# Fewer TensorE waits on GpSimd's transfers in a recurrence followed by an expert layer

## The chip, the cores and the metric

The kernel runs on one core of a Trainium2 chip. The metric is the device time of one execution in microseconds. Before the change three runs took 564.1, 559.63 and 563.5 us, with a median of 563.5 us.

## The reference

Two stages are chained. The first is a gated recurrence over 4 sequences of 5056 steps, with 256 channels each:

```
sig = 1.0 / (1.0 + np.exp(-f_logit))
f = lower_bound + (1.0 - lower_bound) * sig
h = f[:, t] * h + (1 - f[:, t]) * x[:, t]      # for each t; y[:, t] = h
```

The second treats the 20224 rows of y as tokens and sends each to one of 8 experts, the one whose normalized embedding has the largest cosine with the token:

```
logits = xn @ en.T / tau
expert_idx = np.argmax(logits, axis=1)
gate_w = softmax(logits)[chosen expert]
out[mask] = gate_w[mask, None] * (np.maximum(x[mask] @ w1[e], 0.0) @ w2[e])
```

The inner width of an expert is 1024. Input and output are float32, and the kernel multiplies in bf16 inside the experts.

## The kernel before, in words

**Chunks.** The tokens are taken in 40 chunks of 512 (the last has 256). For each chunk SyncE loads f_logit and x (the tiles `fin` and `xin`), TensorE transposes them (L782, L816), ScalarE makes the gate f (L793, L799), and VectorE multiplies (L824) and scans (L840). One or two chunks form a group, of which there are 22. Per group TensorE computes the logits (L945, L949), VectorE finds the expert and the slot of each token, and the rows of h go back to token order in the tile `Yt`.

**Row transfers.** GpSimd then scatters the rows of a group to a buffer in HBM, `XsScratch`, sorted by expert: one indirect transfer for every 128 tokens (`gate_`, L1109), so 4 for a group of one chunk and 8 for a group of two. There are 158 of them.

**Expert tiles.** A tile is 256 rows of one expert (`tile_`). SyncE loads it from `XsScratch`, transposed, into `ys`, and the rows' gates and numbers into `xm`. TensorE multiplies by w1 (L1434, 16 matmuls, two steps of 8) and by w2 (L1482, 16 matmuls, four steps of 4). ScalarE and VectorE apply the ReLU in between (L1455, L1460) and at the end scale the two halves of the result into `osb` (L1497, L1501). GpSimd scatters each half to its place in the output (L1507): 2 output transfers for a tile, 162 for the 81 tiles that run. Ten more tiles stand behind a branch that these inputs don't take. `osb` has 6 buffers, `ys` 6, `Yt` 6 and `xm` 14.

**The order of the work.** Nothing is issued as it is written. `op` records each operation with what it depends on, and `schedule` runs a model of the five engines and fixes the order of each engine's instructions. `resolve` turns dependences into semaphore waits and leaves out those that an engine is already known to have passed. In the model a transfer of GpSimd that is marked `paced` gets one more dependence: the last TensorE step that the model has ended by the time the transfer is issued (`past[-1]`, with `PACE` 0). On the chip GpSimd then waits for that step. All row transfers are marked, and all output transfers but those of the last four tiles. The model also caps the end of a marked transfer at its issue time plus `DMA_FIX`.

GpSimd has one queue of instructions in a fixed order, on which the 16 loads of the expert weights (L762), the row transfers and the output transfers alternate.

Of the kernel before, what the change touches and what calls it, by code (L numbers as in the profile page):

```python
# [34 lines left out]
class Prog:  # L35
# [93 lines left out]
    def schedule(self, first, caps):  # L129
# [43 lines left out]
        while True:  # L173
            best = None
            for e in free:
                while wait[e] and wait[e][0][0] <= free[e]:
                    t, p, i, o = heapq.heappop(wait[e])
                    heapq.heappush(avail[e], (p, i, o))
                if avail[e]:
                    s = free[e]  # L180
                elif wait[e]:
                    s = wait[e][0][0]
# [6 lines left out]
            s, e = best  # L189
# [6 lines left out]
            if soon is not None:  # L196
                wait[e].remove(soon)
                heapq.heapify(wait[e])
                s, p, i, o = soon
            elif avail[e]:  # L200
                p, i, o = heapq.heappop(avail[e])
            else:
                t, p, i, o = heapq.heappop(wait[e])
            gap = s - free[e]
            if e == "pe" and s < self.COLD and gap > self.IDLE:
                room = [(t, q) for q, t in enumerate(frees) if t is not None and t <= s - self.IDLE]
                if room and ready_at(self.warm_on) is not None:
                    t, q = min(room)
                    a = max(t, free[e], ready_at(self.warm_on))
                    n = int((s - a - self.REST) / (self.UNIT * (2 if s < self.COLD else 1)))  # L210
# [29 lines left out]
            if o.dma is not None:  # L240
                bus = max(bus, free[e]) + o.nbytes / self.DMA_RATE
                o.end = max(bus, free[e]) + self.DMA_FIX
                if e == "pool" and o.paced:
                    o.end = min(o.end, free[e] + self.DMA_FIX)
            else:
                o.end = free[e] + self.LAG[e]
# [126 lines left out]
def bass_hgrn_recurrence__then__cosine_router_kernel(  # L373
# [41 lines left out]
    with ExitStack() as es:  # L415
# [106 lines left out]
        def dve(fn, n, fast=False, **k):  # L522
            return op("dve", fn, 75 + n * (0.55 if fast else 1.04), **k)

        def act(fn, n, ptrs=0, **k):
            return op("act", fn, 70 + 0.833 * n + 110 * ptrs, **k)
# [380 lines left out]
        def views(g, hr=None):  # L907
            cc = groups[g]
            K, nb = len(cc), nof(cc[0]) // P
            J = K * nb  # L910
            q = g % R2
            o = bof[g][1] * 8

            def rt_():
                return bank[hr.b][:, 0:392].rearrange("p (b c) -> p b c", b=4)[:, 0:nb, :]

            def Lv():
                return rt_()[:, :, 0:64].rearrange("p b (k e) -> p b k e", k=2)[:, :, 0:K, 0:8]

            def Nv():  # L920
                return rt_()[:, :, 64:98:32][:, :, 0:K]

            def v4(t, o=0):
                return t[:, o * 8 : (o + J) * 8].rearrange("p (b k e) -> p b k e", b=nb, k=K)

            def v3(t, o=0):
                return t[:, o : o + J].rearrange("p (b k) -> p b k", b=nb)

            def bc(t, o=0):
                return v3(t, o).unsqueeze(3).to_broadcast([P, nb, K, 8])  # L930

            return K, nb, J, q, Lv, Nv, v4, v3, bc
# [115 lines left out]
        def gate_(bi):  # L1048

            gg = batches[bi]  # L1050
            JJ = views(gg[0])[2] + (8 if len(gg) > 1 else 0)
            q, y = bi % R2, bi % NY

            n_, y_, t_ = nrm[q][:, 0:JJ], nr2[q][:, 0:JJ], nr3[q][:, 0:JJ]
            ki, ky, kt = ("nrm", q), ("nr2", q), ("nr3", q)
            root(n_, y_, t_, nr4[q][:, 0:JJ], nr5[q][:, 0:JJ], [ki], ky, kt, ("nr4", q), ("nr5", q), 16)
            dve(
                lambda e: e.tensor_scalar(y_, t_, 1e-6, tau, op0=ALU.add, op1=ALU.mult),
                16, r=[kt], w=[ky],
            )  # L1060
            dve(
                lambda e: e.reciprocal(rs[q][:, 0:JJ], nr2[q][:, 0:JJ]), 16,
                r=[("nr2", q)], w=[("rs", q)],
            )
            d3 = df[q][:, 0 : JJ * 8].rearrange("p (j e) -> p j e", e=8)
            dve(
                lambda e: e.tensor_tensor(
                    d3, d3, rs[q][:, 0:JJ].unsqueeze(2).to_broadcast([P, JJ, 8]), ALU.mult
                ),
                128, r=[("rs", q), ("df", q)], w=[("df", q)],  # L1070
            )
            act(
                lambda e: e.activation(exb[q][:, 0:JJ, 0:8], d3, AF.Exp),
                128, r=[("df", q)], w=[("exb", q)],
            )
            dve(
                lambda e: e.tensor_reduce(den[q][:, 0:JJ], exb[q][:, 0:JJ, :], AX.X, ALU.add),
                144, r=[("exb", q)], w=[("den", q)],
            )
            yf = Yt[y][:].bitcast(F32)  # L1080
            for g in gg:
                K, nb, J = views(g)[0:3]
                v3 = views(g)[7]
                o = bof[g][1] * 8
                dve(
                    lambda e, K=K, nb=nb, o=o, v3=v3: e.reciprocal(
                        yf[:, o : o + K * 4, P].rearrange("p (k b) -> p b k", k=K)[:, 0:nb, :],
                        v3(den[q], o),
                    ),
                    8, r=[("den", q)], w=[("Ytg", y)],  # L1090
                )
            K, nb = views(gg[-1])[0:2]
            R = bof[gg[-1]][1] * 8 + (K - 1) * 4 + nb
            dve(
                lambda e: e.tensor_scalar(
                    Yt[y][:].bitcast(I32)[:, 0:R, P + 1], tokf[:, 0:R],
                    float(groups[gg[0]][0] * CH), None, op0=ALU.add,
                ),
                8, r=["tokf"], w=[("Yti", y)], order=[pr.writer[("Ytg", y)]],
            )  # L1100
            for g in gg:
                K, nb, J = views(g)[0:3]
                o = bof[g][1] * 8
                for b in range(nb):
                    for k_ in range(K):
                        j = b * K + k_
                        sc = op(
                            "pool",
                            lambda e, j=o + j, i=o + k_ * 4 + b: e.indirect_dma_start(  # L1109
                                out=Xs[:, :],  # L1110
                                out_offset=bass.IndirectOffsetOnAxis(
                                    ap=sli[y][:, j : j + 1], axis=0
                                ),
                                in_=Yt[y][:].bitcast(I32)[:, i, :],
                                in_offset=None,
                            ),
                            1280, r=[("Yt", y, k_, 0), ("Yt", y, k_, 1), ("Ytg", y), ("Yti", y), ("ytz", y), ("sli", y)],
                            w=[("Xs", g)], dma=f"sc{y}_{k_}", nbytes=100000, chain=False,
                        )
                        sc.paced = True  # L1120


        def update_(u, g, last):
# [188 lines left out]
        NM = N // T + E // 4  # L1312
# [5 lines left out]
        def tile_(j, u, g, n):  # L1318
# [105 lines left out]
            for mp in range(2):  # L1424
# [26 lines left out]
                for m, h in ((2 * mp, hh[0]), (2 * mp + 1, hh[1])):  # L1451
                    o = hT[qh][:, 2 * m : 2 * m + 2, :].rearrange("p f c -> p (f c)")
                    if m % 2 == 0:
                        act(
                            lambda e, o=o, h=h: e.activation(o, bank[h.b][:], AF.Relu), 512,  # L1455
                            h=h, w=[("hT", qh, m)], prio=EVP(pr.prio), tag="mid",
                        )
                    else:
                        dve(
                            lambda e, o=o, h=h: e.tensor_scalar(  # L1460
                                o, bank[h.b][:], 0.0, None, op0=ALU.max
                            ),
# [41 lines left out]
            for s in range(2):  # L1504
                sc = op(
                    "pool",
                    lambda e, s=s: e.indirect_dma_start(  # L1507
                        out=out[:, :],
                        out_offset=bass.IndirectOffsetOnAxis(
                            ap=xm[qx][:, s, 1:2], axis=0  # L1510
                        ),
                        in_=osb[qo][:, s, :],
                        in_offset=None,
                        bounds_check=N - 1,
                        oob_is_err=False,
                    ),
                    1280, r=[("osb", qo, s)] + xk, w=[("out", j, s)], dma=f"od{qo}_{s}",
                    nbytes=170000, prio=OUTP(pr.prio),
                )
                sc.paced = n < NM - 4  # L1520


        last_of = {cc[-1]: g for g, cc in enumerate(groups)}
# [20 lines left out]
        def put(j, n):  # L1544
            u, g = avail[j]
            pr.prio = 10000 + n
            tile_(j, u, g, n)

        for c in range(NCH):
            pr.prio = c  # L1550
            if c >= 2:
                load(c)
            F_(c)
            X_(c)
            Y_(c)
            if c == 0:
                for i in range(2 * E):
                    wload(i, c)
            if c == 1:
                late_constants()  # L1560
            if c in last_of:
                g = last_of[c]
                route_(g)
                bi, gi = bof[g]
                if g == batches[bi][-1]:
                    gate_(bi)
                for u, at in enumerate(ups):
                    if at == g:
                        update_(u, g, u == len(ups) - 1)
# [63 lines left out]
```

How the kernel before makes its waits and increments, by code:

```python
            def part(e, items):  # L347
                for o, waits in items:
                    for key, v in waits:
                        e.wait_ge(sems[key], v)
                    with nc.allow_low_precision(reason="whole numbers below 2**24"):
                        ins = o.fn(e)
                    if o.dma is not None:
                        ins.then_inc(sems[o.dma], 16)
                    elif o.used:
                        ins.then_inc(sems[eng], 1)
```

## Time and profile before

| | |
|---|---|
| runs | 564.1, 559.63, 563.5 us (median 563.5) |
| the profiled execution's own time | 565.46 us |
| its span, first to last instruction | 563.7 us |
| TensorE matmuls | 475.2 us busy, 84% |
| VectorE | 359.5 us, 64% |
| GpSimd | 331.9 us, 59% |
| ScalarE | 321.1 us, 57% |
| mean granted TensorE clock | 0.963 of full speed |

Engines are PE (TensorE matmuls), PEld (TensorE weight loads), DVE (VectorE), ACT (ScalarE), POOL (GpSimd) and SP (SyncE). A line such as L1109 is a line of the kernel. The idle time before an instruction is put down to what ended it; "issue" means that the profile shows nothing that the engine waited for, and "remote" that a semaphore came well after the recorded end of the instruction that sends it. Ends of matmuls are modelled. Landing times of most transfers could not be paired with their issues, so a wait for a landing may appear under another name.

### The profile page before, as it was taken

How to read it: one execution, taken by the hardware profiler on the slowest of the kernel's cores; microseconds unless marked ns; L12 is line 12 of the kernel's file. 1: busy time of each engine (PE TensorE's matmuls, PEld its weight loads, DVE VectorE, ACT ScalarE, POOL GpSimd, SP SyncE). 2: the span in 40 equal slices, each digit the busy share in tenths (PEclk: the TensorE clock that was granted, in tenths of full speed). 3: DMA queues.
4: the chain of work that ended last, by engine and by line, in shares of the span. 5: the costliest groups of instructions: out<-in, count | busy, mean ns of one | idle time of the engine just before them, and what ended most of it. 6: DMA issues, size and time to landing. Idle time of an engine off the chain costs nothing. (4 is left out here: it accounts for less than half of the span.)

```text
span 563.7 us, 12407 instructions
## 1 busy us (share of the span) xinstructions
PE 475.2 (84%) x4106; PEld 382.8 (68%) x4106; DVE 359.5 (64%) x1075; ACT 321.1 (57%) x573; POOL 331.9 (59%) x388
## 2 busy tenths in 40 slices
PE   7796778979798789887887988888988897978994
PEld 4474557757577567656765657777777776867894
DVE  7869978877787667875877876533444343443452
ACT  4878768877787566757776753333333332333342
POOL 6164565655665565564666665656665666655555
PEclk8969988998998889999999999999999999999998
DMA  8999999999999788879896543353343433444422
GB/s 243 302 311 313 318 254 311 287 254 219 206 234 241 202 205 190 238 172 219 221 241 133 117 92 99 113 127 105 100 110 95 110 88 100 106 109 101 106 65 74
DMA packets 119681, 100.49 MB, mean 178 GB/s; under 512 B 96884, under 2 KB 98687, under 8 KB 119616
## 3 DMA queue, kind: packets, MB, share of 16 engines
q1 hardware_dynamic: 101664, 59.38, 42.5%
q0 software_dynamic: 16224, 40.26, 26.2%
q8 instruction: 36, 0.59, 0.5%
q10 hardware_dynamic: 1728, 0.01, 0.2%
q14 instruction: 29, 0.24, 0.2%
HBM read 59.21 MB, written 32.93 MB: 163 GB/s over the span
## 5 line engine op out<-in xcount | busy, mean ns | idle before, releaser
L1507 POOL DMA_INDIRECT out_dram<-osb,xm x162 | 160.7, 992 | 107.6 <-issue 34.0
L1109 POOL DMA_INDIRECT XsScratch<-Yt,sli x158 | 152.2, 963 | 105.6 <-issue 26.6
L1434 PE MATMUL bank<-ys,wall 128*128 128x256 bf16 (+1 forms) x1392 | 174.4, 271 | 19.1 <-issue 13.4
L1482 PE MATMUL bank<-wall,hT 128*128 x1296 | 172.8, 274 | 15.0 <-issue 12.6
L1460 DVE TENSOR_SCALAR hT<-bank 128x512 bf16<-128x512 f32 x162 | 108.4, 684 | 100.8 <-remote 46.0
L1434 PEld LDWEIGHTS bank<-ys,wall 128*128 x1392 | 147.5, 145 | 34.9 <-issue 24.7
L1455 ACT ACTIVATE hT<-bank 128x512 bf16<-128x512 f32 x162 | 94.0, 597 | 114.1 <-remote 49.5
L1482 PEld LDWEIGHTS bank<-wall,hT 128*128 128x128 bf16 x1296 | 124.4, 98 | 42.9 <-issue 23.0
L840 DVE TENSOR_TENSOR_SCAN hb<-fg,hb,bank 128x512 f32<-128x512 f32 (+4 forms) x78 | 95.9, 1236 | 0.1
L1501 DVE TENSOR_SCALAR osb<-bank,xm 128x256 f32<-128x256 f32 x81 | 38.8, 479 | 59.7 <-ACT osb L1497 32.6
L1497 ACT ACTIVATE osb<-bank,xm 128x256 f32<-128x256 f32 x81 | 38.4, 475 | 59.7 <-remote 17.4
L816 PE MATMUL bank<-ident,xin 128*128 128x128 f32 x316 | 53.2, 294 | 22.7 <-ACT fg L799 12.9
L799 ACT ACTIVATE fg<-th,cs 128x512 f32<-128x512 f32 (+1 forms) x80 | 64.4, 812 | 1.4 <-DVE cs L627 0.2
L816 PEld LDWEIGHTS bank<-ident,xin 128*128 128x128 f32 x316 | 37.7, 149 | 34.6 <-ACT fg L799 16.9
L824 DVE SCALAR_TENSOR_TENSOR bank<-fg,bank 128x512 f32<-128x512 f32 (+1 forms) x80 | 54.1, 680 | 9.6 <-PE bank L816 6.8
L793 ACT ACTIVATE th<-bank 128x512 f32<-128x512 f32 (+1 forms) x80 | 46.3, 592 | 22.7 <-PE bank L782 14.2
L782 PE MATMUL bank<-ident,fin 128*128 128x128 f32 x316 | 53.5, 300 | 4.5 <-DMA fin<-in_f_logit_dram 2.0
L782 PEld LDWEIGHTS bank<-ident,fin 128*128 128x128 f32 x316 | 40.4, 155 | 12.2 <-issue 4.5
L852 ACT ACTIVATE sq<-hb 128x1024 f32<-128x1024 f32 (+1 forms) x40 | 41.8, 1045 | 2.0 <-DVE hb L840 1.6
L945 PE MATMUL bank<-hb,eT 128*8 128x512 f32 (+1 forms) x160 | 41.7, 599 | 0.3 <-issue 0.3
L949 PE MATMUL bank<-sq,onesf 128*1 128x512 f32 (+1 forms) x160 | 41.5, 597 | 0.0
L861 ACT ACTIVATE hbf<-hb 128x512 bf16<-128x512 f32 x50 | 31.4, 629 | 4.7 <-DVE hb L840 4.2
(139 smaller groups left out, 305.3 us busy)
## 6 DMA issues: line engine op xcount, KB each, us to landing
fin<-in_f_logit_dram SPq DMA_DIRECT2D x39, 512.0 KB
xin<-in_x_dram SPq DMA_DIRECT2D x39, 512.0 KB
wall<-in_moe_w_dram POOLq DMA_DIRECT2D x16, 512.0 KB, 10.6
out_dram<-osb,xm POOLq DMA_INDIRECT x162
XsScratch<-Yt,sli POOLq DMA_INDIRECT x158
ys<-XsScratch SPq DMA_TRANSPOSE x81
xm<-XsScratch SPq DMA_DIRECT2D x75, 2.0 KB
osb<-XsScratch SPq DMA_DIRECT2D x6, 136.0 KB
```

The source lines that it names most:

```text
L782: i = e.transpose(bank[h.b][:, b : nb * P : nb], fin[q][:, b, dh * P : (dh + 1) * P], ident[:],)
L793: lambda e, dh=dh, h=h: e.activation(th[dh][:, 0:n], bank[h.b][:, 0:n], AF.Tanh, scale=0.5),
L799: lambda e, dh=dh: e.activation(fg[c % 2][:, dh, 0:n], th[dh][:, 0:n], AF.Identity, bias=cs[:, dh, 0:1], scale=cs[:, dh, 1:2],),
L816: i = e.transpose(bank[h.b][:, b : nb * P : nb], xin[q][:, b, dh * P : (dh + 1) * P], ident[:],)
L824: lambda e, dh=dh, h=h: e.scalar_tensor_tensor(out=bank[h.b][:, 0:n], in0=fg[c % 2][:, dh, 0:n], scalar=1.0, in1=bank[h.b][:, 0:n], op0=AL ...
L840: lambda e, dh=dh, s0=s0, s1=s1, init=init, h=h: e.tensor_tensor_scan(hb[c % NH][:, dh, s0:s1], fg[c % 2][:, dh, s0:s1], bank[h.b][:, s0:s ...
L1109: lambda e, j=o + j, i=o + k_ * 4 + b: e.indirect_dma_start(out=Xs[:, :], out_offset=bass.IndirectOffsetOnAxis(ap=sli[y][:, j : j + 1], axis=0
L1434: i = e.matmul(bank[hh[f // 2].b][:, at : at + R_], wall[:, bass.ds(a1[j, s][(4 * mp + f) * DT + kt] - WA - WREV, 2 * FT * P),].bitcast(BF ...
L1455: lambda e, o=o, h=h: e.activation(o, bank[h.b][:], AF.Relu), 512,
L1460: lambda e, o=o, h=h: e.tensor_scalar(o, bank[h.b][:], 0.0, None, op0=ALU.max),
L1482: i = e.matmul(po(s), hT[qh][:, kf, s * P : (s + 1) * P], wall[:, bass.ds(a2[j, s if last else 0][kf] - WA, 2 * D)].bitcast(BF16), start=( ...
L1507: lambda e, s=s: e.indirect_dma_start(out=out[:, :], out_offset=bass.IndirectOffsetOnAxis(ap=xm[qx][:, s, 1:2], axis=0), in_=osb[qo][:, s, :],
```

## The change

Two marks are set for fewer transfers. Of a group's row transfers, only every fourth (`j % 4 == 0`) is paced now; of a tile's two output transfers, only the first (`s == 0`). The cap on the end of a transfer in the model now goes by the name of its semaphore (`sc` for rows, `od` for outputs) instead of the mark, so that it still holds for all of them.

```
-                if e == "pool" and o.paced:
+                if e == "pool" and o.dma[:2] in ("sc", "od"):
                     o.end = min(o.end, free[e] + self.DMA_FIX)
...
-                        sc.paced = True
+                        sc.paced = j % 4 == 0
...
-                sc.paced = n < NM - 4
+                sc.paced = s == 0 and n < NM - 4
```

On every engine the instructions stand in the same order as before; only waits differ. Of the 320 row and output transfers that run, 283 waited for a TensorE semaphore (149 of the 158 row transfers, 134 of the 162 output transfers); now 116 do (40 and 76). Two pieces of GpSimd's queue show it. In brackets are the semaphores that an instruction waits for: `s_pe`, `s_dve` and `s_act` are those of TensorE, VectorE and ScalarE, `s_w8` that of a weight load, `s_xm5` that of a tile's gates. A row with `-` is before, with `+` after.

The first piece is GpSimd's queue in the first 100 us, with row transfers of two groups between weight loads:

```order
 L762 DMA wall<-in_moe_w_dram 128x2x1024 [waits s_w8]
 L1109 DMA XsScratch<-Yt,sli 164096x136 [waits s_pe,s_dve]
-L1109 DMA XsScratch<-Yt,sli 164096x136 [waits s_pe] x3
+L1109 DMA XsScratch<-Yt,sli 164096x136 x3
 L762 DMA wall<-in_moe_w_dram 128x2048 [waits s_w9]
-L1109 DMA XsScratch<-Yt,sli 164096x136 [waits s_pe] x4
+L1109 DMA XsScratch<-Yt,sli 164096x136 [waits s_pe]
+L1109 DMA XsScratch<-Yt,sli 164096x136 x3
 L762 DMA wall<-in_moe_w_dram 128x2x1024 [waits s_w10]
```

The first transfer of four keeps its wait, and the other three follow it without one.

The second piece is GpSimd's queue where tiles and chunks run together, after the change alone:

```order
+L1507 DMA out_dram<-osb,xm 20224x256 [waits s_xm5,s_pe,s_act]
+L1507 DMA out_dram<-osb,xm 20224x256 [waits s_dve]
+L1109 DMA XsScratch<-Yt,sli 164096x136 [waits s_pe]
+L1109 DMA XsScratch<-Yt,sli 164096x136
+L1507 DMA out_dram<-osb,xm 20224x256 [waits s_xm6,s_pe,s_act]
+L1507 DMA out_dram<-osb,xm 20224x256 [waits s_dve]
+L1109 DMA XsScratch<-Yt,sli 164096x136 x2
```

The second output transfer of a tile waits for its data alone (`s_dve`), and of the row transfers one in four waits. The longest run of transfers without a TensorE wait is now 4.

## Rows read from the trace of the kernel before

**Rows 1.** The page: busy time of TensorE and GpSimd, slices, and queue q0.

```profile
PE 475.2 (84%) x4106; PEld 382.8 (68%) x4106; DVE 359.5 (64%) x1075; ACT 321.1 (57%) x573; POOL 331.9 (59%) x388
...
q0 software_dynamic: 16224, 40.26, 26.2%
```

**Rows 2.** Busy time by stage: start to end, busy us (instructions) by engine, clock, DMA, GB/s.

```profile
core 0: us, PE busy (x) PEld busy (x) DVE busy (x) ACT busy (x) POOL busy (x), PEclk, DMA share, GB/s
0.00:100.00 100.00, 77.77 (x586) 56.81 (x590) 82.43 (x279) 74.34 (x119) 54.36 (x104) 0.88 1.01 294
100.00:350.00 250.00, 213.66 (x1876) 165.36 (x1869) 189.71 (x633) 172.25 (x306) 149.70 (x154) 0.97 0.82 198
350.00:553.00 203.00, 180.00 (x1617) 157.54 (x1616) 84.76 (x159) 72.57 (x146) 121.92 (x125) 1.00 0.41 103
```

**Rows 3.** TensorE's waits, whole span: what it waited for, us, times, longest us.

```profile
PE bank L1434 <- issue: 13.4, 29, 2.3
PE bank L816 <- ACT fg L799: 12.9, 10, 2.8
PE bank L1482 <- issue: 12.6, 24, 1.2
...
PE bank L1434 <- DVE osb L1501: 2.4, 3, 1.6
PE bank L816 <- DMA xin<-in_x_dram: 2.0, 1, 2.0
PE bank L782 <- DMA fin<-in_f_logit_dram: 2.0, 3, 1.6
```

**Rows 4.** The groups of both kinds of transfer: busy us, mean ns, idle before.

```profile
L1507 POOL DMA_INDIRECT out_dram<-osb,xm x162 | 160.7, 992 | 107.6 <-issue 34.0 <-DVE hT L1460 26.1 <-ACT osb L1497 7.2
L1109 POOL DMA_INDIRECT XsScratch<-Yt,sli x158 | 152.2, 963 | 105.6 <-issue 26.6 <-PE bank L782 13.1 <-PE bank L1434 13.1
```

**Rows 5.** Line L1109 alone: shortest, median and longest of its transfers in ns.

```profile
L1109 POOL DMA_INDIRECT XsScratch<-Yt,sli x158: 952/959/1059, 27.5 to 482.6; - x158
```

**Rows 6.** Row transfers alone by stage (stretch, POOL busy and count, clock, DMA, GB/s).

```profile
0.00:100.00 100.00, 35.95 (x37) 0.88 1.01 294
100.00:350.00 250.00, 88.36 (x92) 0.97 0.82 198
350.00:553.00 203.00, 27.87 (x29) 1.00 0.41 103
```

**Rows 7.** GpSimd in order of time: start us, us, instruction, idle before it.

```profile
257.18 1.00 POOL L1507 DMA_INDIRECT out_dram<-osb,xm  x1 [0.30 <-issue]
258.48 0.96 POOL L1109 DMA_INDIRECT XsScratch<-Yt,sli  x1 [0.30 <-issue]
259.75 0.95 POOL L1109 DMA_INDIRECT XsScratch<-Yt,sli  x1 [0.30 <-issue]
262.36 0.96 POOL L1109 DMA_INDIRECT XsScratch<-Yt,sli  x1 [1.66 <-PE bank L1434]
263.62 0.95 POOL L1109 DMA_INDIRECT XsScratch<-Yt,sli  x1 [0.30 <-issue]
```

**Rows 8.** SyncE's waits from 350 us on: what it waited for.

```profile
SPq L1329 <- remote: 25.8, 9, 4.3
...
SPq L1329 <- PE bank L1482: 17.5, 9, 2.6
SPq L1329 <- PE bank L1434: 11.7, 6, 3.3
```

**Rows 9.** ScalarE and GpSimd at the end of the span, in order of time.

```profile
552.53 0.48 ACT L1497 ACTIVATE osb<-bank,xm 128x256 f32<-128x256 f32 x1 [2.44 <-PE bank L1434]
...
553.80 0.98 POOL L1507 DMA_INDIRECT out_dram<-osb,xm  x1 [2.27 <-DVE osb L1501]
555.09 0.99 POOL L1507 DMA_INDIRECT out_dram<-osb,xm  x1 [0.30 <-issue]
...
560.26 0.98 POOL L1507 DMA_INDIRECT out_dram<-osb,xm  x1 [0.30 <-issue]
```

**Rows 10.** TensorE's waits from 350 us on.

```profile
PE bank L1482 <- issue: 10.8, 21, 1.2
PE bank L1434 <- issue: 9.8, 24, 1.1
...
PE bank L1434 <- DVE hT L1460: 0.9, 2, 0.5
```

**Rows 11.** GpSimd, then TensorE, around one of these stalls, in order of time.

```profile
465.18 0.99 POOL L1507 DMA_INDIRECT out_dram<-osb,xm  x1 [0.30 <-issue]
466.47 0.98 POOL L1507 DMA_INDIRECT out_dram<-osb,xm  x1 [0.30 <-issue]
468.97 0.96 POOL L1109 DMA_INDIRECT XsScratch<-Yt,sli  x1 [1.51 <-remote]
...
466.32 0.60 PE L1482 MATMUL bank<-wall,hT 128*128 x4
467.32 0.27 PE L1482 MATMUL bank<-wall,hT 128*128 x1 [0.39 <-issue]
468.01 0.38 PE L1482 MATMUL bank<-wall,hT 128*128 x2 [0.43 <-issue]
```

## The prediction

> **What bounds the kernel now.** I read the busy times first, by stage. TensorE's matmuls are busy for 475.2 of 563.7 us, more than any other engine [rows 1], and from 350 us to 553 us for 180.0 of 203.0 us, while VectorE, ScalarE and all transfers are near or under half [rows 2]. The reader should see there that GpSimd is busy for 121.92 us in the same 203 us: it has room.
>
> Next come TensorE's own waits [rows 3]. The largest are stalls with no cause in the profile ("issue", 13.4 and 12.6 us) and 12.9 us for ScalarE's gate in the chunks. Three waits are for anything that a transfer of any queue could carry: 2.0 us for x, 2.0 us for f_logit, and 2.4 us behind VectorE's write of `osb`, a tile that an output transfer frees. No row of TensorE's waits names a row transfer or an output transfer. SyncE, which loads the tiles that the row transfers fill, waits in the late stage for TensorE, 17.5 and 11.7 us [rows 8]; another 25.8 us stand under "remote", a semaphore that came later than the modelled end of its sender. That too is a TensorE signal as far as can be told, and no landing of a row transfer stands in the list.
>
> Then GpSimd itself [rows 4, 7]. A transfer holds it for 0.963 or 0.992 us, and one that is free to go follows the one before after 0.30 us, which is a period of about 1.27 us. Where a wait binds, the gap is longer: 1.66 us before the row transfer at 262.36. So the removed waits do bind now, and not all are empty.
>
> So the bound is TensorE, in the late stage nearly alone, and GpSimd follows it.
>
> **The change part by part.** The order of the instructions stays on all engines, so the change is waits alone: 167 TensorE waits fewer on GpSimd (283 less 116), none added. Nothing is moved past anything.
>
> *What GpSimd gains.* The idle time before row and output transfers is 105.6 + 107.6 = 213.2 us [rows 4]. Of that, 320 x 0.30 = 96 us is the unavoidable gap; the other 117 us or so is waiting, and part of it goes. But the first transfer of four and the first of a tile keep their wait, the longest run without one is 4, and the gap left out is mostly 0.7 to 1.4 us (1.66 less 0.30 at 262.36), so a single transfer starts some 1 to 4 us sooner. It lies beside TensorE's work; if that cover were gone, up to those 117 us would matter.
>
> *What an earlier row transfer is worth.* It would matter if SyncE waited for it. By its waits it does not [rows 8], so I take 0. A gain is left possible all the same, since landings are badly paired in this trace: were a tenth of the 25.8 us under "remote" such waits and TensorE short of that tile, 2.6 us. The ends are 0 and -2.6.
>
> *What an earlier output transfer is worth.* It frees `osb` sooner. The nearest row is TensorE's 2.4 us behind the write of `osb` [rows 3]. The ends are 0 and -2.4 us; I take -1.0, because the write itself, 0.48 us for a half tile [rows 9] in each of the three times, stays.
>
> *The end of the span.* ScalarE's scaling at 552.53 ends at 553.01, the next output transfer starts at 553.80, and five more follow in steps of 1.29 us, to 561.24 [rows 9]. These belong to tiles that were not paced before either. Worth 0; it would take an earlier end of TensorE to move it.
>
> *What the burst costs.* Three of four row transfers now leave sooner than the plan had them, beside the loads of x, f_logit and the tiles. The queue that GpSimd feeds took 26.2% of the 16 engines' span [rows 1], or 147.7 us, for 338 transfers (162, 158, 16 weight loads and 2 small ones), which is 0.44 us each. Three brought forward hold a load behind them for at most 1.3 us. The ends are 0, since TensorE hardly waits for a load, and 13 us, if each of the nine or ten bursts of four in the first 100 us (37 row transfers [rows 6]), where the transfer engines are full (1.01) [rows 2], delayed a load that TensorE then lacks. I take +0.5, close to the low end, because the row nearest to it is the 4.0 us of waits for x and f_logit in the whole span [rows 3], and an eighth more of that is 0.5. The Trainium skill, DMA: Bandwidth & Descriptors, section Issuing engines are not separate DMA queues, says that transfers started by any engine run on the same 16 engines and interleave. By it earlier row transfers must come out of the loads' share; the trace agrees that the engines are full at first (1.01), and this speaks against the change.
>
> *Making descriptors in a burst.* Row transfers take 952 to 1059 ns with a median of 959 over a span in which VectorE is busy 64% [rows 1, 5], so none is stretched to speak of; I take 0. The Trainium skill, SBUF — State Buffer, section SBUF: two separate sides, warns that VectorE in certain modes locks GpSimd out while it writes descriptors, which would stretch a burst. No row here shows it, and by the 1059 ns it could add 0.1 us to a transfer.
>
> *Sum.* 565.46 - 1.0 + 0.5 = 565.0 us against the profiled execution's own time. That execution lies 2.0 us above the median of 563.5, so against the runs the sum gives **563.0 us**, no change that could be measured. A change is told from none here at about 1%, that is below 557.9 or above 569.1; the three runs alone spread over 4.5 us.
>
> **The rivals.**
>
> *Faster: the late stalls belong to GpSimd's timing.* In the last 214 us TensorE loses 10.8 + 9.8 = 20.6 us in 45 stalls with no wait in the program [rows 10], as between 466.32 and 468.01, where matmuls that need nothing come 0.7 us apart [rows 11]. If they come from something that the transfers' timing sets, and an evener stream takes a third away, 6.9 us go: 563.0 - 6.9 = 556.1 us. For it: GpSimd ran several transfers in a row just before (465.18, 466.47) [rows 11]. Against it: GpSimd is held by a stall in TensorE anyway, so the rows would look like this either way, and the stage before 350 us has the same rate of transfers with fewer of these stalls (26.0 us in all, of which 20.6 are late) [rows 3, 10]. Chance 0.16.
>
> *Slower: bursts in the first 100 us.* Place: the chunks up to 100 us, where the transfer engines are full at 1.01 and 294 GB/s and weights are loaded too [rows 2]. Three row transfers go 1 to 3 us earlier, and the load of x or f_logit behind them comes up to 1.3 us later. Price: half of the 13 us above, 6.5 us, 569.5 us. It decides from the point where a load has less than 1.3 us to spare in more than about half of the bursts. For it: the full engines, and four waits for such loads already (4.0 us). Against it: x and f_logit have three buffers each, and TensorE waited only those four times. Chance 0.08.
>
> *Slower: longer stalls late.* The same 45 stalls, longer by a third because output transfers now come in closer pairs: 563.0 + 6.9 = 569.9 us. The evidence is that of the first rival with the other sign. Chance 0.07.
>
> *The change does nothing.* The kept wait, or the data, holds each run of four just as long. The time is 563.5 us; inside the forecast, and not told from it.
>
> **How the numbers follow.** Forecast, including the last case: 0.69; its own range is 559.5 to 567, the spread of the runs shown with the bounds of -2.4 and -2.6 and part of the burst's cost. The faster rival gets 0.16, the two slower ones 0.15. The predicted time is 563.0. To leave out no more than 2 in 10, the range takes in the faster rival at 556.1 and the two slower ones at 569.5 and just short of 569.9: 555.5 to 569.8. Faster by over 1%: 0.16; within 1%: 0.69; slower by over 1%: 0.15.
>
> **What would show it.** In the profile after, GpSimd's busy time stays near 332 us and its gaps before the second to fourth row transfer and before the second output transfer fall to 0.30 us, with longer gaps before the ones that still wait. TensorE's busy time stays near 475 us, its waits for x and f_logit near 4 us, its "issue" stalls after 350 us near 20 us. The last run of six output transfers starts 0.8 us after a scaling and has the same 1.29 us steps. I am wrong if "issue" falls or rises by over 5 us from 350 us on (first and third rival), if waits for x and f_logit pass 8 us (second), or if a wait for a row transfer's landing held TensorE all along without being named.

## The result, and the profile after

The changed kernel took 600.41 us (median of 6 runs, 592.47 to 607.6), the kernel before beside it 561.76 us (6 runs, 559.63 to 564.1). The ratio is 1.0645, with a 95% interval of 1.0586 to 1.0703: **slower by 6.5%**, where no measurable change was forecast. One run of after, 607.6 us, fell in a slower state of the chip and isn't in the ratio, which for that reason lies below that of the two medians.

The profiled execution of after took 599.74 us, its span is 597.9 us, 34.2 us more than before, and the mean granted clock is 0.925 (0.963 before). The page's line of busy times, to be held against [rows 1]:

```profile
PE 494.0 (83%) x4106; PEld 394.4 (66%) x4106; DVE 361.0 (60%) x1075; ACT 325.4 (54%) x573; POOL 332.6 (56%) x388
```

All engines ran the same instructions. GpSimd, VectorE and ScalarE were busy for nearly what they were before, but TensorE's matmuls for 18.8 us longer, and TensorE stood idle for 15.4 us longer (597.9 - 494.0 = 103.9, before 563.7 - 475.2 = 88.5). The two make the 34.2 us.

GpSimd's groups of transfers, the view of [rows 4], and the spread of the row transfers, the view of [rows 5]:

```profile
L1507 POOL DMA_INDIRECT out_dram<-osb,xm x162 | 160.8, 993 | 155.5 <-DVE osb L1501 34.1 <-issue 27.1 <-DVE hT L1460 22.6
L1109 POOL DMA_INDIRECT XsScratch<-Yt,sli x158 | 152.7, 966 | 93.0 <-issue 39.4 <-PE bank L1434 8.6 <-PE bank L782 7.3
```
```profile
L1109 POOL DMA_INDIRECT XsScratch<-Yt,sli x158: 956/962/1072, 26.7 to 514.7; - x158
```

A transfer lasts as long as before. The idle time moved: less before row transfers (93.0 after 105.6), much more before output transfers (155.5 after 107.6). GpSimd reaches them sooner and then waits for data that come later.

TensorE's waits over the whole span, against [rows 3]:

```profile
PE bank L816 <- ACT fg L799: 18.0, 13, 4.0
PE bank L1434 <- issue: 13.4, 25, 1.2
PE bank L1482 <- issue: 10.2, 20, 1.0
PE bank L816 <- issue: 5.9, 5, 3.7
...
PE bank L1434 <- DVE osb L1501: 4.6, 3, 3.7
PE bank L1434 <- DVE hT L1460: 4.2, 5, 2.3
```
```profile
PE bank L816 <- DMA xin<-in_x_dram: 1.2, 1, 1.2
```

The waits for ScalarE and VectorE grew and became longer singly (4.0 us where 2.8 was the longest); those for loads shrank. Something holds up all the compute engines. What it is stands in the waits of ScalarE and VectorE, which the prediction did not read. Before first, two rows of ScalarE and one of VectorE:

```profile
ACT hT L1455 <- remote: 49.5, 13, 5.7
ACT osb L1497 <- remote: 17.4, 6, 5.5
```
```profile
DVE hT L1460 <- remote: 46.0, 14, 5.2
```

The same waits after, with the next row of each engine:

```profile
ACT hT L1455 <- remote: 41.9, 11, 6.6
ACT osb L1497 <- remote: 23.4, 8, 4.3
ACT th L793 <- remote: 13.4, 4, 5.4
```
```profile
DVE hT L1460 <- remote: 39.4, 11, 6.5
DVE rmax L976 <- remote: 12.1, 3, 4.7
```

All these waits are for TensorE's semaphore, which came well after the matmuls that send it are recorded as ended. In the kernel before, ScalarE already spent 73 us in rows of this kind and VectorE 46 us, in single waits of up to 5.7 us. After, it is 87 and 56 us: the rows of `hT` are smaller, those of other steps have grown or are new.

A stretch between two semaphore events of TensorE in which its signals don't come is called a silence here. Of TensorE's idle time between its first and its last matmul (80.1 us before, 95.1 us after), 55.8 us before and 72.0 us after lie in silences of over 2 us. So what TensorE stood longer, it stood in silences.

**One place in both.** The same six transfers and the same ScalarE step. Start and duration in us, then the idle time before. First GpSimd and ScalarE before:

```profile
267.62 0.99 POOL L1507 DMA_INDIRECT out_dram<-osb,xm  x1 [1.77 <-DVE bank L824]
268.91 1.00 POOL L1507 DMA_INDIRECT out_dram<-osb,xm  x1 [0.30 <-issue]
270.22 0.97 POOL L1109 DMA_INDIRECT XsScratch<-Yt,sli  x1 [0.31 <-issue]
271.49 0.95 POOL L1109 DMA_INDIRECT XsScratch<-Yt,sli  x1 [0.30 <-PE bank L967]
273.54 0.95 POOL L1109 DMA_INDIRECT XsScratch<-Yt,sli  x1 [1.09 <-PE bank L1434]
274.80 0.95 POOL L1109 DMA_INDIRECT XsScratch<-Yt,sli  x1 [0.30 <-issue]
```
```profile
273.35 0.47 ACT L1497 ACTIVATE osb<-bank,xm 128x256 f32<-128x256 f32 x1 [1.86 <-PE bank L1434]
```

Then the same after, with TensorE's steps:

```profile
280.09 0.99 POOL L1507 DMA_INDIRECT out_dram<-osb,xm  x1 [1.79 <-DVE bank L824]
281.39 1.00 POOL L1507 DMA_INDIRECT out_dram<-osb,xm  x1 [0.30 <-issue]
282.70 0.97 POOL L1109 DMA_INDIRECT XsScratch<-Yt,sli  x1 [0.30 <-issue]
283.97 0.96 POOL L1109 DMA_INDIRECT XsScratch<-Yt,sli  x1 [0.30 <-issue]
285.24 0.96 POOL L1109 DMA_INDIRECT XsScratch<-Yt,sli  x1 [0.30 <-issue]
286.50 0.96 POOL L1109 DMA_INDIRECT XsScratch<-Yt,sli  x1 [0.30 <-issue]
```
```profile
288.82 0.47 ACT L1497 ACTIVATE osb<-bank,xm 128x256 f32<-128x256 f32 x1 [4.30 <-remote]
```
```profile
283.07 0.60 PE L1482 MATMUL bank<-wall,hT 128*128 x4
283.88 0.66 PE L782 MATMUL bank<-ident,fin 128*128 128x128 f32 x4 [0.20 <-DVE nr L1058]
284.63 1.09 PE L1434 MATMUL bank<-ys,wall 128*128 128x256 bf16 x8
285.56 0.60 PE L816 MATMUL bank<-ident,xin 128*128 128x128 f32 x4
289.87 1.39 PE L1434 MATMUL bank<-ys,wall 128*128 128x256 bf16 x7 [3.71 <-DVE osb L1501]
```

Before, the wait of the fifth transfer left a gap of 1.09 us after the fourth, and ScalarE's step came 0.9 us after that fourth transfer had ended (272.44). After, six transfers stand in one row up to 287.46. The matmuls that ScalarE needs (L1482) are recorded at 283.07, yet it starts only at 288.82, and TensorE itself, out of work that needs nobody, is idle for 3.71 us. The step lags by 15.5 us (288.82 - 273.35), 3.0 us more than the transfers ahead of it (280.09 - 267.62 = 12.5): that much is lost in this one place.

The clock follows such a stop. TensorE, granted clock and DMA in windows of after, columns as in [rows 2]:

```profile
284.00:288.00 4.00, 2.06 (x16) 1.58 (x16) 0.77 (x4) 0.52 (x1) 2.86 (x3) 1.00 0.90 288
288.00:291.00 3.00, 1.13 (x7) 1.01 (x8) 2.30 (x11) 2.18 (x5) 0.00 (x0) 0.88 0.39 122
291.00:294.00 3.00, 3.00 (x18) 2.23 (x16) 1.94 (x6) 2.59 (x5) 1.36 (x2) 0.55 0.65 128
294.00:297.00 3.00, 3.00 (x38) 2.91 (x37) 1.98 (x7) 2.17 (x4) 1.68 (x3) 1.00 0.85 145
```

After a stretch of 7 us in which TensorE was busy for 3.2 us, the clock is granted at 0.55, near its lower level of 1.2 GHz: 18 matmuls start in 3 us, then 38. Up to TensorE's last matmul the stretches at half clock add up to 37.5 us before and 85.3 us after, and TensorE was busy for 33.2 and 75.7 us of them. Half of the 42.5 us more is an estimate of 21 us, enough for the 18.8 us that the matmuls took longer. How much of the loss is clock differs from run to run: when the changed kernel ran again (after_2, 601.11 us), TensorE was busy for 486.5 us, only 11.3 more than before.

### The profile page after: what moved, and what is told of

It reads as the page before. It is cut to its first block and busy times, and to the rows that moved or that the text cites. A ratio compares the mean times of both kernels' runs of the same rounds, so it can differ in the third digit from the quotient of the medians.

```text
span 597.9 us, 12355 instructions
## 1 busy us (share of the span) xinstructions
PE 494.0 (83%) x4106; PEld 394.4 (66%) x4106; DVE 361.0 (60%) x1075; ACT 325.4 (54%) x573; POOL 332.6 (56%) x388
## 5 line engine op out<-in xcount | busy, mean ns | idle before, releaser
L1507 POOL DMA_INDIRECT out_dram<-osb,xm x162 | 160.8, 993 | 155.5 <-DVE osb L1501 34.1
L1434 PE MATMUL bank<-ys,wall 128*128 128x256 bf16 (+1 forms) x1392 | 182.4, 279 | 30.0 <-issue 13.4
L1109 POOL DMA_INDIRECT XsScratch<-Yt,sli x158 | 152.7, 966 | 93.0 <-issue 39.4
L1482 PE MATMUL bank<-wall,hT 128*128 x1296 | 180.0, 283 | 15.0 <-issue 10.2
L1434 PEld LDWEIGHTS bank<-ys,wall 128*128 x1392 | 152.7, 147 | 47.9 <-issue 21.8
L1482 PEld LDWEIGHTS bank<-wall,hT 128*128 128x128 bf16 x1296 | 128.1, 101 | 45.9 <-issue 20.0
L816 PE MATMUL bank<-ident,xin 128*128 128x128 f32 x316 | 54.5, 299 | 27.1 <-ACT fg L799 18.0
L816 PEld LDWEIGHTS bank<-ident,xin 128*128 128x128 f32 x316 | 38.6, 152 | 39.2 <-ACT fg L799 25.8
L945 PE MATMUL bank<-hb,eT 128*8 128x512 f32 (+1 forms) x160 | 44.5, 633 | 2.8 <-ACT sq L852 2.7
L949 PE MATMUL bank<-sq,onesf 128*1 128x512 f32 (+1 forms) x160 | 44.4, 631 | 0.0
```

The lines of the kernel that those rows point to most:

```text
L816: i = e.transpose(bank[h.b][:, b : nb * P : nb], xin[q][:, b, dh * P : (dh + 1) * P], ident[:],)
L1109: lambda e, j=o + j, i=o + k_ * 4 + b: e.indirect_dma_start(out=Xs[:, :], out_offset=bass.IndirectOffsetOnAxis(ap=sli[y][:, j : j + 1], axis=0
L1434: i = e.matmul(bank[hh[f // 2].b][:, at : at + R_], wall[:, bass.ds(a1[j, s][(4 * mp + f) * DT + kt] - WA - WREV, 2 * FT * P),].bitcast(BF ...
L1482: i = e.matmul(po(s), hT[qh][:, kf, s * P : (s + 1) * P], wall[:, bass.ds(a2[j, s if last else 0][kf] - WA, 2 * D)].bitcast(BF16), start=( ...
L1507: lambda e, s=s: e.indirect_dma_start(out=out[:, :], out_offset=bass.IndirectOffsetOnAxis(ap=xm[qx][:, s, 1:2], axis=0), in_=osb[qo][:, s, :],
```

## The experiments

All kernels below keep the order of the instructions of the kernel before, apart from added memsets. They ran on five chips. On one, the kernel before took 471.8 us; on the four others 563 to 571 (561.76 in the first comparison). That is the first finding.

### Which waits, on a chip that turned out to be another one

rows_only undoes the output half of the change (`sc.paced = n < NM - 4` again), outs_only the row half (`sc.paced = True`), no_pace sets both marks to False. gap is the changed kernel plus a GpSimd memset of a tile of 128x590 bf16 (`gap`) ahead of each of these transfers that has no TensorE wait:

```
+    if o.dma is None or o.late or o.dma[:2] not in ("sc", "od"):
+        return []
+    if not (not any(k == 'pe' for k, v in waits)):
+        return []
...
+    e.memset(self.gap[:], 0.0).then_inc(self.sems["gap"], 1)
```

**rows_only.** 

> Only the row transfers lose waits (one of four is paced); the output transfers are paced as before. Theory, runs: GpSimd's back-to-back runs of four and more transfers hold TensorE up, and the row transfers, which stand four to eight in a row in the queue, make most of the long runs, so most of the 38.7 us come: 582 to 595 us. Rival, outputs: output transfers take more of the transfer engines each, and the earlier second one is what hurts: within 1% of before, 557 to 568 us.

**outs_only.** 

> Only the output transfers lose waits (the second of a tile isn't paced); the row transfers are all paced as before. Theory, runs: a wait of a row transfer stands between nearly all pairs, runs stay short, and less than half of the loss comes: 563 to 580 us. Rival, outputs: nearly the whole loss, 590 to 601 us.

**no_pace.** 

> No transfer waits for a TensorE step; only data and buffers hold them. Theory, runs: runs grow further, and the time goes above that of the change: 605 to 630 us. Rival, the change's waits fall badly (a kept wait that delays a whole run behind it): without any, back to 560 to 575 us.

**gap.** 

> The changed kernel, with a GpSimd memset of 590 columns (about 0.6 us, into a tile that nothing reads) ahead of each row or output transfer that doesn't wait for TensorE. No wait for TensorE is added. Theory, runs (spacing): the transfers then stand about 2.1 us apart instead of 1.27, and most of the loss goes: 562 to 578 us. Rival, synchronisation: what the removed waits did was to tie a transfer to TensorE's progress, and distance doesn't replace that: 592 to 605 us.

Measured beside 471.83 us: rows_only 0.999 (0.9948 to 1.0031), outs_only 0.9998 (0.9959 to 1.0038), no_pace 0.9974 (0.9945 to 1.0004), gap 1.1624 (1.1547 to 1.17). None of the expected times fits, since none reckoned with this chip. Without any TensorE wait (no_pace) GpSimd issues long stretches without a pause, and nobody minds; GpSimd and ScalarE from the trace:

```profile
291.78 0.97 POOL L1109 DMA_INDIRECT XsScratch<-Yt,sli  x1 [0.30 <-issue]
293.05 0.96 POOL L1109 DMA_INDIRECT XsScratch<-Yt,sli  x1 [0.30 <-ACT osb L1497]
294.32 0.96 POOL L1109 DMA_INDIRECT XsScratch<-Yt,sli  x1 [0.30 <-DVE hT L1460]
295.58 1.00 POOL L1507 DMA_INDIRECT out_dram<-osb,xm  x1 [0.30 <-issue]
```
```profile
ACT hT L1455 <- PE bank L1434: 58.5, 107, 1.3
```

Runs there, with gaps under 0.5 us, are of 110 and 141 transfers (247 in rows_only), no wait of ScalarE or VectorE is "remote", and ScalarE's longest wait for L1434 is 1.3 us. TensorE, busy for 436.8 of 468.8 us (93%), is nearest to being the bound, and no TensorE wait for `osb` is left to speak of. GpSimd is close behind: in rows_only its transfers stood idle for 57.9 + 55.4 = 113.3 us, of which 320 gaps of 0.30 us are 96, so it has some 17 us to spare in a span of 468.3. That is why the memsets of gap (204 of 0.625 us, 127.4 us) lengthen the time by 77 us and make GpSimd the bound. ScalarE and TensorE then wait for its output transfers:

```profile
ACT osb L1497 <- DMA out_dram<-osb,xm: 76.5, 30, 8.1
```
```profile
PE bank L1434 <- DVE osb L1501: 24.9, 14, 6.3
```

So a run of transfers does not by itself hold TensorE up; on the other chips, as the next runs show, it does.

### The same on the other chips

**after_2** (the changed kernel again). 

> The changed kernel itself once more, beside the kernel before. The last four runs stood beside a kernel before of 471.8 us, not 561.8, and in their traces no semaphore of TensorE came late ('remote' was gone from the waits). Theory, chip: what the change costs depends on late TensorE semaphores that some chips or sessions show; where the kernel before takes about 472 us, the change is within 1% of it (468 to 476 us), where it takes about 562 us, the change takes 593 to 608 us. Rival: the change costs about 38 us either way (505 to 515 us beside 472).

**rows_2** (as rows_only). 

> Only the row transfers lose waits, as in the earlier run of this kernel, for a second session. Where the kernel before takes about 472 us: the same as before, 468 to 476 us. Where it takes about 562 us: by the theory of runs most of the loss, 582 to 595 us; by the rival that output transfers make it, 557 to 568 us.

Beside 562.96 us: after_2 1.0627 (1.0561 to 1.0693), rows_2 1.0629 (1.0577 to 1.0682). The loss comes back on this chip, and the row transfers alone make all of it, where the theory had given them most of it (582 to 595 us; 599.33 measured).

**outs_2** (as outs_only). 

> Only the output transfers lose waits; all row transfers are paced. Where the kernel before takes about 562 us (there rows_only took 599 us, the whole loss): theory, a loss only where a wait between row transfers is gone: 558 to 568 us. Rival, any TensorE wait that is taken from GpSimd costs, in proportion (58 of 167): 570 to 580 us. Where the kernel before takes about 472 us: 469 to 476 us.

**no_pace_2** (as no_pace). 

> No transfer waits for a TensorE step. Where the kernel before takes about 562 us: theory, runs (TensorE's signals stay away while GpSimd issues transfers back to back and come about 1 us after a run's end): runs grow, 605 to 640 us. Rival, the four waits in ten that are left fall badly: 560 to 580 us. Where the kernel before takes about 472 us: 468 to 474 us.

**gap_2** (as gap). 

> The changed kernel with a GpSimd memset of 590 columns (0.625 us) ahead of each of the 204 row and output transfers that don't wait for TensorE. GpSimd alone then needs about 549 us, as the run beside 472 us showed, so less than that can't come. Where the kernel before takes about 562 us: theory, runs: with pauses of 0.9 us TensorE's signals come through, 550 to 580 us, below the change's 600. Rival, synchronisation: distance doesn't replace the wait for TensorE: 600 us or more.

**gap3** (no_pace, with the memset if `sent % 3 == 0`). 

> No transfer waits for a TensorE step; instead a GpSimd memset of 590 columns stands ahead of every third row or output transfer, so that at most three follow each other closely. GpSimd's own work is 332 + 107 x 0.8 us and 0.3 us a transfer, about 500 us. Where the kernel before takes about 562 us: theory, runs (silence of TensorE's signals had a median of 2.2 to 2.3 us at runs of three, 3.6 to 5.8 us at five and six): 545 to 580 us, and well below no_pace. Rival, synchronisation: as no_pace, above 600 us. Where the kernel before takes about 472 us: 495 to 515 us, by GpSimd's work alone.

Beside 568.33 us: outs_2 1.0042 (1.0004 to 1.008), no_pace_2 1.1176 (1.1101 to 1.1251), gap_2 0.9992 (0.9957 to 1.0026), gap3 609.28 us (four runs, 599.99 to 611.61), 1.072 by the medians (no interval). The waits for late signals in no_pace_2, ScalarE and VectorE:

```profile
ACT hT L1455 <- remote: 57.9, 14, 6.9
```
```profile
DVE hT L1460 <- remote: 52.5, 13, 6.7
```

and in gap_2, with a piece of its GpSimd stream:

```profile
ACT hT L1455 <- remote: 26.0, 15, 4.1
```
```profile
DVE hT L1460 <- remote: 22.9, 13, 3.9
```
```profile
280.90 0.98 POOL L1109 DMA_INDIRECT XsScratch<-Yt,sli  x1 [0.17 <-ACT hbf L861]
282.18 0.99 POOL L1507 DMA_INDIRECT out_dram<-osb,xm  x1 [0.30 <-issue]
283.14 0.64 POOL L1642 MEMSET gapt<- 128x590 bf16 x1
283.94 1.00 POOL L1507 DMA_INDIRECT out_dram<-osb,xm  x1 [0.17 <-issue]
```

outs_2, no_pace_2 and gap_2 came out as the theory of runs had it, measured against this kernel before. gap_2 has as few TensorE waits as the changed kernel, GpSimd is busier than ever (455.9 us), and yet the time is that of the kernel before: pauses of about 0.8 us ahead of 204 transfers do what the 167 waits did. So the removed waits can be replaced by distance, and it isn't that GpSimd is busy. (The changed kernel itself wasn't run on this chip; no_pace_2 shows that the chip has the effect.)

gap_2 still has 116 TensorE waits, though, and gap3, which has none, fell into the range of the rival, synchronisation (above 600 us), and outside its theory's (545 to 580 us). A pause ahead of every third transfer takes back only 25 of the 66 us that no_pace_2 lost. before_gap3, further down, has the same memsets and all 283 waits, and in both no run is longer than three (57 runs of three there, 67 in gap3), yet it takes 0.996 of the kernel before. At like spacing the waits are thus worth some 7%, and distance is not all that counts. One reading is that a wait holds GpSimd until TensorE's signal has come, however late, and a pause of 0.8 us doesn't: in gap3 the signals come back 1.2 us after the end of a run of three (median). That is not shown, since no run has a pause ahead of every transfer and no TensorE wait.

### Data, or the issuing

out_thin is the kernel before with output transfers of 32 bytes a row into a scratch tensor; the output stays unwritten:

```
-                        out=out[:, :],
+                        out=thin[:, :],                      # [N, 8] float32 in HBM
...
-                        in_=osb[qo][:, s, :],
+                        in_=osb[qo][:, s, 0:8],
```

**out_thin.** 

> The kernel before, with every output transfer writing 8 columns of a row (32 bytes) to a scratch tensor instead of 256 columns (1 KB) to the output, which stays unwritten. Number and place of the transfers, their 128 rows and their waits are unchanged. Where the kernel before takes 562 to 568 us: theory A, the transfers' data (41 MB of queue q0 become half) hold TensorE's signals up: the silences behind runs of output transfers go, and with them 10 us or more: ratio 0.95 to 0.98. Theory B, the issuing itself (GpSimd makes 128 rows' descriptors back to back, whatever they carry): ratio 0.99 to 1.01, and silences of 4 to 6 us behind runs of five and six stay. Where the kernel before takes about 472 us, GpSimd's issuing is the bound: 0.99 to 1.01 by both.

Measured 0.9948 (0.9903 to 0.9993) beside 570.65 us, and the silences stay (of VectorE's waits):

```profile
DVE hT L1460 <- remote: 39.4, 13, 5.5
```

This is what theory B had for the output transfers: with a thirty-second of their data the late signals stay, so it is not the amount of their data that holds TensorE's signals up. That it is the issuing itself is not shown by this. The same for row transfers wasn't tried, since the tiles are loaded from what they write.

### Number of waits, or runs; and where

every2 is the changed kernel with `sc.paced = j % 2 == 0`. rows_early and rows_late keep all output waits and take three of four row waits from the groups of the first 20 chunks, or from the later ones (`j % 4 == 0 or groups[g][0] >= 20`, and `< 20`).

**every2.** 

> The changed kernel with every second row transfer paced instead of every fourth. Where the kernel before takes 562 to 568 us: theory, runs: between outs_2 (1.004, all rows paced) and the change (1.063), 1.015 to 1.045. Rival, a threshold (only runs of four and more row transfers cost): as outs_2, 0.995 to 1.01. Where the kernel before takes about 472 us: 0.99 to 1.005.

**rows_early.** 

> One of four row transfers is paced for the groups of the first 20 chunks (up to about 210 us), all of them for later groups; outputs paced as before. Theory, runs hurt where TensorE is on a chain with ScalarE, VectorE and the chunks: half of the loss lies here, ratio 1.02 to 1.045. Rival, only the late stage counts, where TensorE alone is the bound: 0.995 to 1.015. Beside a kernel before of about 472 us: 0.99 to 1.005.

**rows_late.** 

> The other half: all row transfers of the first 20 chunks paced, one of four for the later groups (210 to 480 us). Theory: the other half of the loss, 1.02 to 1.04. Rival (late stage alone): the whole, 1.05 to 1.065. Beside a kernel before of about 472 us: 0.99 to 1.005.

**before_gap3** (the kernel before with the memset ahead of every third transfer). 

> The kernel before with all its waits, and a GpSimd memset of 590 columns (0.625 us) ahead of every third row or output transfer besides. Theory, its own runs of four to six cost it time too: 0.96 to 0.99. Rival, what is left in it lies beside other work, and the memsets only delay transfers: 0.995 to 1.02. Beside a kernel before of about 472 us, where GpSimd's issuing is the bound: 1.05 to 1.10.

every2 1.0083 (1.0024 to 1.0141) beside 570.65 us; rows_early 1.0276 (1.0198 to 1.0355), rows_late 1.0299 (1.0239 to 1.0359), before_gap3 0.9956 (0.9913 to 0.9999), all beside 569.8 us. Set side by side, with the transfers that still wait for TensorE, the sum of the silences over 3 us, and TensorE's idle time that lies in silences over 2 us. Both are worked out from the times of TensorE's semaphore events in each trace (some events may be missing, and a silence can also be a time in which TensorE has nothing to send, so they are measures, not times):

| kernel | row waits | output waits | ratio | TensorE busy us | silences, us | idle in silences, us |
|---|---|---|---|---|---|---|
| before | 149 | 134 | 1 | 475.2 | 211 | 56 |
| before_gap3 | 149 | 134 | 0.996 | 473.1 | 195 | 56 |
| gap_2 | 40 | 76 | 0.999 | 478.0 | 157 | 46 |
| outs_2 | 155 | 73 | 1.004 | 474.3 | 219 | 56 |
| every2 | 79 | 76 | 1.008 | 475.3 | 229 | 60 |
| rows_early | 93 | 134 | 1.028 | 477.6 | 245 | 70 |
| rows_late | 95 | 137 | 1.030 | 482.9 | 232 | 67 |
| rows_2 | 39 | 137 | 1.063 | 494.1 | 241 | 75 |
| after | 40 | 76 | 1.0645 | 494.0 | 238 | 72 |
| gap3 | 0 | 0 | 1.072 | 494.4 | 222 | 73 |
| no_pace_2 | 0 | 0 | 1.118 | 499.3 | 305 | 88 |

The sum of the silences alone doesn't order the kernels (gap3 and every2 stand against it), nor do ScalarE's and VectorE's waits under "remote" (112 us together in rows_2, 119 before); the idle time of TensorE inside the silences does, nearly. What TensorE is busy longer is its clock: take off half of the busy time that fell at half clock, and 456 to 462 us are left for every kernel of the table (an estimate).

every2 has fewer waits than rows_late and costs a quarter of it, so the number of waits doesn't decide. The time of every2 fell into the range of the rival, a threshold, and below that of the theory of runs (1.015 to 1.045). What counts among these kernels is how many transfers follow each other unwaited: one behind a waited one costs little, three cost 6%. The two halves of the span add up (2.8% + 3.0% against 6.3%), so there is no one place; both expectations of a half hold, and the rival of the late stage falls. before_gap3 lies in the range of its rival, at the edge of no difference: the runs that the kernel before has left cost little that such pauses could take back.

## Why the prediction was wrong, point by point

- **What bounds the kernel.** That TensorE is the bound, with GpSimd at 59%, held as far as busy times go. The reading stopped at TensorE's own waits. The 25.8 us under "remote" in [rows 8] were taken as TensorE's and put aside; the same word stood with 49.5 and 46.0 us in the longest rows of ScalarE's and VectorE's waits.
- **What GpSimd gains.** The gaps did fall to 0.30 us, and GpSimd's busy time stayed (332.6). The longest run without a TensorE wait is 4 but for the last nine transfers, which have none (the last eight before). That the gaps lay beside TensorE's work and so had no value is **the step that failed**: with those gaps gone TensorE's signals came later, and the change cost 6.5%; with pauses put in their place (gap_2) it cost nothing (0.999). [Rows 7] show the gap of 1.66 us that was written off. TensorE's busy time, forecast to stay near 475 us, rose to 494.0.
- **Earlier row and output transfers.** Worth nothing, where 0 and -1.0 us were taken: no wait of TensorE names their landing, and GpSimd waited longer before its output transfers (155.5 us). The wait behind `osb` rose from 2.4 to 4.6 us instead of falling by 1.0.
- **The burst's cost.** Sized at 0.5 us, and looked for in the wrong place, the transfer engines. The wait for x fell from 2.0 to 1.2 us and f_logit left the list. The Trainium skill, DMA: Bandwidth & Descriptors, section Issuing engines are not separate DMA queues, says that transfers started by ScalarE, SyncE or GpSimd run on the same 16 DMA engines and interleave. That the loads would lose share by it was the prediction's inference; no wait of TensorE shows any effect of it. The price of the closer transfers was 34.2 us of span, and it came by another way, the late signals.
- **Making descriptors in a burst.** The row transfers kept their length (956 to 1072 ns), as said. Their effect on others wasn't asked.
- **The end of the span.** The steps of 1.29 us stayed and nothing was lost there, as said; the last run has four transfers, not six.
- **The late "issue" stalls.** Forecast to stay near 20 us; from 350 us on they are 11.0 + 10.0 us, against 9.8 + 10.8 in [rows 10]. So neither this sign of being wrong nor that of the loads came. The rival that let them grow by 6.9 us when transfers stand closer had the right cause, closer transfers, but put it on stalls that didn't change, late in the span, at a fifth of the size, with a chance of 0.07. (By [rows 2] GpSimd ran 258 instructions in the 350 us before this stage and 125 in its 203 us, so the rate was a fifth higher before it, not the same.) The rival of the first 100 us falls too: by the traces the same step lags by only 3 us at 94 us, and then by 13 at 200, 28 at 347 and 34 at the end, and the waits for loads shrank.
- **[Rows 11]** lie at the end of a run of five transfers (461.32 to 467.45 us), with TensorE out of step beside it. The argument that GpSimd "is held by a stall in TensorE anyway" took one direction without weighing the other: TensorE's signals, silent for 5.7 us, came back 1.2 us after the run had ended, at 468.7.

That the loss comes from transfers which GpSimd issues closely, without waits between them, is shown by rows_2, every2 and no_pace_2, which take away more waits or fewer, and by gap_2, which puts pauses in place of the removed ones. That it reaches the time through late signals rests on the traces: TensorE's idle time in silences, and the half clock, make up the difference. How far a wait does more than a pause is open (gap3). Through which part of the chip the transfers hold TensorE's signals up is not shown; nor why one chip of five is free of it. The changed kernel itself wasn't run on that one; its two halves and the kernel without any wait cost nothing there.

## What to carry to other kernels

A wait that only delays an engine off the path may be spacing what that engine does to others: before removing it, read the waits of all engines for signals that come late, and see whether they stand behind runs of that engine's work. Where one is to be loosened, leave it at every second item first, and time it. A variant that is worse on one chip can be equal on another that lacks the effect, so look at the time of the kernel before in each session.

## What the runs showed of the hardware

- The same kernel took 471.8 us on one chip and 562 to 571 on the others. The traces differ in TensorE's late signals: on that chip no wait of ScalarE or VectorE was "remote" (rows_only, outs_only, no_pace), the silences over 3 us add up to 14 to 21 us instead of 211, and TensorE was busy for 94% of the span (rows_only). An output transfer took GpSimd 994 ns there and 992 on the other.
- During a silence of over 4 us in the kernel before, starts of matmuls are mostly still recorded for 2 to 5 us before TensorE stands still, and signals of steps that lie apart arrive together (three within 0.15 us at 288.8 in after). Counted by run length before: the silence around the end of a run has a median of 1.2 us for single transfers, 2.2 for two and three, 3.0 for four, 5.2 for five, and ends 0.5 to 1.3 us after the run. In rows_only, on the chip without late signals, it is 0.7 to 1.0 us for runs of two to four, and 0.9 us at the end of a run of 247.
- A stop of TensorE can cost twice, since the clock can fall to half after it: up to the last matmul there are 8 such stretches before and 16 after. That was over half of the loss in the first trace of after (18.8 of 34.2 us), but less when it ran again (11.3 us).
